# Linear attention, gated MLP and top-1 MoE on one core: the products with the state as eight half-column matmuls in place of four whole ones

## The chip, the core and the metric

The kernel runs on one core of a Trainium2 chip, in f32. The metric is the time of one execution on the device, in microseconds. The median of three runs of the kernel before is 538.46 us (538.27 to 538.58).

## What is computed

Three stages follow one another: a linear attention with a decaying state, a gated MLP, and a mixture of eight experts of which each token takes one. The change lies in the first.

```python
q, k, v: (2, 8, 768, 64)     # batch, heads, tokens, width; lam: one decay for each head
for b in range(nb):          # blocks of tokens, in order
    intra = einsum('bhic,bhjc->bhij', qb, kb) * Dmask      # scores, weighed by the decay
    intra = einsum('bhij,bhjd->bhid', intra, vb)
    inter = einsum('bhid,bhde->bhie', qb * lam_pow, kv_state)
    out[:, :, sl] = intra + inter
    kv_state = lam_block * kv_state + einsum('bhsd,bhse->bhde', kb * rev_pow, vb)
x = moe2(moe(out))
```

## The kernel before

The attention works on 12 tiles (n = 0 to 11, NT = 12), each 128 tokens of one of the two batches, in turn: even n are batch 0, odd n batch 1. The eight heads stand as four pairs (NPAIR = 4); the two heads of a pair (z = 0, 1) take partitions 0 to 63 and 64 to 127.

TensorE's instructions for a tile are four blocks, written out in order by the loop at L836:

- `from_state(n)`, for n of 2 and more: four matmuls (L792), one for each pair. The stationary operand is the pair's state, 128x128, in which only the two 64x64 blocks on the diagonal hold values and the others are zero. The moving operand is `qs`, the queries times powers of the decay, 128x128. The product starts the sum in the output bank. It waits for `qs` (POOL), for the state (VectorE) and for `xl_ready`, with which VectorE gives the bank free.
- `to_state(n)`, for n from 1 to 9: eight matmuls (L808) with the decayed keys `kd` as 128x64 stationary, the output in partitions z*64 to z*64+63.
- `scores(n + 1)`: eight matmuls (L783), 64 rows by 128 columns.
- `within(n)`: eight matmuls (L819) with 128x64 stationary (values) and 128 moving columns (`pt`, the weighed scores). They add to the output bank and write partitions z*64 to z*64+63, pair by pair.

Around them: the SyncE queue loads a tile's input in two transfers (L456, L457) once `within(n - 4)` is done. POOL makes `kd` (L590), `qs` (L601) and `faded`, the decayed state (L606). VectorE weighs the scores into `pt` (L1667), splits the output into a high and a low part (`xh` by ScalarE at L1246, `xl` by VectorE at L1607), and adds to the state (L1686). From n = 8 on it also makes a difference of tiles, `xt` (L1737). ScalarE copies the output as `xt` and `xh`, and splits the first MLP weights (`gvh`). In tile 11 VectorE makes `gvl` (L1693) straight behind the weighing; the first product of the MLP, `gate_val(0, 0)` (L857), waits for it. From there TensorE runs the MLP (L857, L865, L889, L932) and the experts (L1159, L1169).

In the profile each f32 matmul of the source is two weight loads and two matmuls, so the four matmuls of `from_state` are x8 and the eight of the others x16.

Of the kernel before, what the change touches and what calls it, by code (L numbers as in the profile page):

```python
# [20 lines left out]
B, H, S, D = 2, 8, 768, 64  # L21
# [3 lines left out]
CH = 128  # L25
# [69 lines left out]
def bass_linear_attention_mlp_moe(nc, attn_in, lam_rows, mlp_w, router_w, expert_w, out):  # L95
    ctx = ExitStack()
    with ctx:
        def sb(name, shape, dt=F32, stack=ctx):
            return stack.enter_context(nc.sbuf_tensor(name, shape, dt))
# [62 lines left out]
        qs = [sb(f"qs{i}", [P, NPAIR, CH], F32, region1) for i in range(2)]  # L162
        kd = [sb(f"kd{i}", [P, H, D], F32, region1) for i in range(2)]
        pt = [[sb(f"pt{i}_{z}", [P, NPAIR, CH], F32, region1) for z in range(2)] for i in range(2)]
        state = [sb(f"state{b}", [P, NPAIR, P], F32, region1) for b in range(B)]
# [65 lines left out]
        bank = ctx.enter_context(nc.psum_tensor("bank", [P, 8, 512], F32))  # L231
# [122 lines left out]
        S_BANK, O_BANK, K_BANK = (0, 4), (2, 6), (3, 7)  # L354
# [85 lines left out]
        def read_passes(eng):  # L440
            eng.wait_ge(slots_ready, 1)
            return eng.value_load(passes[0:1, 0:1], min_val=1, max_val=MAXPASS)
# [328 lines left out]
        def _(pe):  # L771
            mm = nc.tensor.matmul
# [14 lines left out]
            def from_state(n):  # L787
                pe.wait_ge(qs_ready, n - 1)
                pe.wait_ge(state_ready, 2 * (n - 1))
                pe.wait_ge(xl_ready, n - 1)  # L790
                for a in range(NPAIR):
                    last = mm(bank[:, O_BANK[n % 2], a * CH:(a + 1) * CH], state[n % 2][:, a, :], qs[n % 2][:, a, :],  # L792
                              start=(a == 0), stop=False, skip_group_check=True)
                last.then_inc(inter_done, 1)

            def to_state(n):
# [39 lines left out]
            for n in range(NT):  # L836
                if n >= 2:
                    from_state(n)
                if 1 <= n < LAST_STATE:
                    to_state(n)  # L840
                if 1 <= n < NT - 1:
                    scores(n + 1)
                within(n)
# [390 lines left out]
            n = read_passes(pe)  # L1234
# [947 lines left out]
```

## Time and profile before

| what | value |
|---|---|
| median of three runs | 538.46 us (538.27 to 538.58) |
| the profiled execution | 538.59 us |
| its span, first to last instruction | 536.9 us |
| TensorE's granted clock, mean | 0.998 |
| TensorE busy | 528.0 us, 98% |
| VectorE, ScalarE, POOL busy | 352.4, 247.4, 75.4 us |
| attention, as far as the first product of the MLP | 0 to 51 us |

The profile is of one execution. Busy time of TensorE counts overlapping records, so the length of a block of matmuls is read from the start of the block to the start of the next one, or from the chain of work that ended last.

### The profile page before, as it was taken

What the parts mean: (1) busy time and instruction counts of PE and PEld (TensorE: products, weight loads), DVE (VectorE), ACT (ScalarE), POOL (GpSimd) and SP (SyncE); (2) the same over time, 40 slices, a digit from 0 to 9 for tenths busy, and PEclk for the clock granted to TensorE, in tenths of its full rate; (3) what the DMA queues carried; (4) which work ended last, traced back from release to release, by engine and by line L of the source; (5) the groups of instructions that cost most, each with busy time, mean ns of one, the idle gap of its engine ahead of it and who ended that gap; (6) DMA issues with size and microseconds to landing.
All of it is one profiled execution on the core that took longest, in us unless ns stands there. A gap on an engine that the chain in (4) does not pass through costs nothing.

```text
span 536.9 us, 8448 instructions
## 1 busy us (share of the span) xinstructions
PE 528.0 (98%) x3195; PEld 448.0 (83%) x3195; DVE 352.4 (66%) x609; ACT 247.4 (46%) x414; POOL 75.4 (14%) x94
## 2 busy tenths in 40 slices
PE   8999999999999999999999999999999999999995
PEld 7888888888888887887888888778999999999994
DVE  7779888795865647644556676567676666766620
ACT  4225465645353424442435444366555555555521
POOL 4992000000000000010000120023021130311001
PEclk9999999999999999999999999999999999999999
DMA  8987404132130304546253656256675666655000
GB/s 291 326 268 280 155 20 157 38 120 104 54 117 21 107 13 153 197 123 248 85 159 106 228 173 247 90 190 238 223 258 211 205 221 225 216 196 175 0 28 36
DMA packets 22280, 84.55 MB, mean 158 GB/s; under 512 B 3804, under 2 KB 3804, under 8 KB 18656
## 3 DMA queue, kind: packets, MB, share of 16 engines
q1 hardware_dynamic: 17376, 71.35, 38.4%
q0 software_dynamic: 3712, 10.54, 5.5%
q10 hardware_dynamic: 1152, 2.13, 1.0%
q8 instruction: 25, 0.41, 0.3%
q14 instruction: 15, 0.12, 0.1%
HBM read 75.59 MB, written 10.53 MB: 160 GB/s over the span
## 4 chain that ended last, share of the span: by engine, by line
PE 95%; issue 1%; DMA 1%; POOL 1%; SPq 0%; POOLq 0%; ACT 0%; DVE 0%
PE bank L932 18%; PE bank L857 16%; PE bank L1159 14%; PE bank L1169 12%; PE bank L865 12%; PE bank L889 6%; PE bank L1073 2%; PE bank L1092 2%; PE bank L783 2%; PE bank L792 2%; PE bank L819 2%; PE bank L1148 1%; PE bank L808 1%; DMA stages<-attn_in 1%; PE bank L959 1%
## 5 line engine op out<-in xcount | busy, mean ns | idle before, releaser
L1607 DVE TENSOR_TENSOR ewl<-stages,ewh 128x1024 fp32r<-128x1024 f32 x50 | 60.8, 1223 | 16.4 <-ACT ewh L1246 15.9
L1246 ACT ACTIVATE ewh<-stages 128x1024 fp32r<-128x1024 f32 x50 | 52.3, 1056 | 0.2 <-DMA stages<-expert_w 0.2
L1552 ACT ACTIVATE ehh<-bank 128x256 fp32r<-128x256 f32 x48 | 18.5, 385 | 58.0 <-PE bank L1159 57.9
L636 POOL DMA_DIRECT2D stages<-expert_w x8 | 4.6, 574 | 260.7 <-DVE more_hl L1607 185.1
L1169 PE MATMUL bank<-ewl,ehh 128*128 128x512 f32 x96 | 37.8, 394 | 0.0
L1169 PE MATMUL bank<-ewh,ehl 128*128 128x512 f32 x96 | 37.7, 392 | 0.0
L1169 PE MATMUL bank<-ewh,ehh 128*128 128x512 f32 x96 | 37.5, 390 | 0.0
L1159 PEld LDWEIGHTS bank<-exh,ewh 128*128 128x128 f32 x224 | 33.2, 188 | 3.6
L1159 PE MATMUL bank<-exh,ewh 128*128 128x256 f32 x224 | 36.0, 283 | 0.0
L2090 DVE SCALAR_TENSOR_TENSOR ehl<-bank,ehh 128x256 fp32r<-128x256 f32 x48 | 20.3, 422 | 23.8 <-ACT ehh L1552 23.7
L1159 PE MATMUL bank<-exl,ewh 128*128 128x256 f32 x224 | 34.8, 278 | 0.0
L1159 PE MATMUL bank<-exh,ewl 128*128 128x256 f32 x224 | 34.7, 277 | 0.0
L857 PE MATMUL bank<-xh,gvh 128*128 128x512 f32 x128 | 34.4, 391 | 0.0
L857 PE MATMUL bank<-xh,gvl 128*128 128x512 f32 x128 | 34.2, 389 | 0.0
L857 PE MATMUL bank<-xl,gvh 128*128 128x512 f32 x128 | 34.2, 389 | 0.0
L651 POOL DMA_INDIRECT gx<-x_rows,idx x15 | 16.1, 1076 | 106.8 <-issue 86.6
L1159 PEld LDWEIGHTS bank<-exl,ewh 128*128 128x128 f32 x224 | 30.2, 189 | 0.0
L1159 PEld LDWEIGHTS bank<-exh,ewl 128*128 128x128 f32 x224 | 29.7, 188 | 0.0
L1246 ACT ACTIVATE c<-bank 128x512 f32<-128x512 f32 x30 | 17.9, 596 | 24.3 <-PE bank L932 24.3
L865 PE MATMUL bank<-hh,woh 128*128 128x512 f32 x72 | 28.7, 399 | 0.0
L857 PEld LDWEIGHTS bank<-xl,gvh 128*128 128x128 f32 x128 | 24.0, 188 | 5.0
L857 PEld LDWEIGHTS bank<-xh,gvl 128*128 128x128 f32 x128 | 24.0, 188 | 5.0
(291 smaller groups left out, 1248.4 us busy)
## 6 DMA issues: line engine op xcount, KB each, us to landing
stages<-expert_w SPq DMA_DIRECT2D x21, 1024.0 KB, 4.9
stages<-mlp_w SPq DMA_DIRECT2D x24, 768.0 KB, 4.5
stages<-attn_in SPq DMA_DIRECT2D x18, 512.0 KB, 5.4
stage<-expert_w SPq DMA_DIRECT2D x7, 1024.0 KB
stages<-expert_w POOLq DMA_DIRECT2D x8, 512.0 KB, 5.5
stage<-attn_in SPq DMA_DIRECT2D x6, 512.0 KB, 5.6
held<-c SPq DMA_DIRECT2D x12, 256.0 KB, 2.0
stages<-held SPq DMA_DIRECT2D x12, 256.0 KB, 2.8
```

What stands on the lines that cost most here:

```text
L651: nc.gpsimd.indirect_dma_start(out=dst[:, :], out_offset=None, in_=src, in_offset=bass.IndirectOffsetOnAxis(ap=at, axis=0), bounds_check=l ...
L783: last = mm(bank[:, S_BANK[n % 2] + z, a * CH:(a + 1) * CH], kt[z * D:(z + 1) * D, a, :], qt[z * D:(z + 1) * D, a, :], start=True, stop=True)
L857: last = mm(bank[:, where, :], wt[:, k, :], (xh, xl)[x][:, k, g * GT:(g + 1) * GT], start=(at == 0), stop=(at == 3 * KD - 1))
L865: last = mm(bank[:, d, :], (woh, wol)[w][wo][:, d * P:(d + 1) * P], (hh, hl)[x][h][:, :], start=(f == 0 and n == 0), stop=True, skip_group ...
L889: last = mm(bank[:, d, :], (woh, wol)[w][j % 3 + 1][:, d * P:(d + 1) * P], (hh, hl)[x][j % 3 + 1][:, :], start=(j == 0 and n == 0), stop=True,
L932: last = mm(where, mix(i, w)[:, n * KH * P + k * P:n * KH * P + (k + 1) * P], moving[i][x][:, k, :], start=(first and at == 0), stop=(at = ...
L1159: last = mm(bank[:, H_BANK + f % 2, 0:CAP], expert_bufs(par)[w][:, f, k * P:(k + 1) * P], (exh, exl)[z][par][:, k, :], start=(at == 0), st ...
L1169: last = mm(bank[:, Y_BANK + t, 0:DM], (ehh, ehl)[z][f % 2][:, t * P:(t + 1) * P], expert_bufs(par)[w][:, f, KD * P:], start=(f == 0 and n ...
L1246: return nc.scalar.activation(dst, src, ACT.Copy)
L1552: nc.scalar.activation(ehh[f % 2][:, :], bank[:, H_BANK + f % 2, 0:CAP], ACT.Relu).then_inc(ehh_ready, 1)
L1607: V.tensor_tensor(dst, src, high.bitcast(F32), ALU.subtract).then_inc(inc, 1)
L2090: V.scalar_tensor_tensor(out=ehl[f % 2][:, :], in0=bank[:, H_BANK + f % 2, 0:CAP], scalar=0.0, in1=ehh[f % 2][:, :].bitcast(F32), op0=ALU.max,
```

## The change

`from_state` makes each product as two matmuls. Half z takes columns z*64 to z*64+63 of the pair's state as a 128x64 stationary and writes partitions z*64 to z*64+63 of the output bank. The moving operand is the same 128 columns of `qs` for both. Start flags, waits and the semaphore on the last matmul are as before, and so are the results: each half still takes all 128 rows, zeros included.

```diff
                 for a in range(NPAIR):
-                    last = mm(bank[:, O_BANK[n % 2], a * CH:(a + 1) * CH], state[n % 2][:, a, :], qs[n % 2][:, a, :],
-                              start=(a == 0), stop=False, skip_group_check=True)
+                    for z in range(2):
+                        part = slice(z * D, (z + 1) * D)
+                        last = mm(bank[part, O_BANK[n % 2], a * CH:(a + 1) * CH], state[n % 2][:, a, part],
+                                  qs[n % 2][:, a, :], start=(a == 0), stop=False, skip_group_check=True)
                 last.then_inc(inter_done, 1)
```

## Rows read from the trace of the kernel before

**Rows 1.** The page: TensorE's busy time, and the chain's shares by engine
```profile
PE 528.0 (98%) x3195; PEld 448.0 (83%) x3195; DVE 352.4 (66%) x609; ACT 247.4 (46%) x414; POOL 75.4 (14%) x94
...
PE 95%; issue 1%; DMA 1%; POOL 1%; SPq 0%; POOLq 0%; ACT 0%; DVE 0%
```

**Rows 2.** The chain in order of time: start us, us, what; attention and beyond
```profile
26.59 1.09 PE bank L792 x8
...
29.39 1.02 PE bank L819 x16
...
51.00 21.98 PE bank L857 x96
```

**Rows 3.** Waits of PE, whole run: engine line, releaser: us, times, longest
```profile
PE bank L792 <- POOL qs L601: 0.5, 1, 0.5
PE bank L1202 <- DVE ewl L2106: 0.3, 1, 0.3
```

**Rows 4.** Single lines of PE: ns min/median/max, first and last start, forms
```profile
L792 PE MATMUL bank<-qs,state x80: 275/275/377, 15.1 to 49.7; 128*128 128x128 f32 x80
...
L819 PE MATMUL bank<-pt,stages x144: 272/273/323, 11.0 to 48.6; 128*64 128x128 f32 x144
```

**Rows 5.** Timeline of PE, a tile in the middle: start us, us, instructions
```profile
23.79 0.69 PE L808 MATMUL bank<-stages,kd 128*64 128x64 f32 x16
24.40 1.16 PE L783 MATMUL bank<-stages 64*128 64x128 f32 x16
25.50 1.09 PE L819 MATMUL bank<-pt,stages 128*64 128x128 f32 x16
26.52 1.16 PE L792 MATMUL bank<-qs,state 128*128 128x128 f32 x8
```

**Rows 6.** Timeline of PE, the first tiles, where L808 and L819 are neighbours
```profile
10.96 1.05 PE L819 MATMUL bank<-pt,stages 128*64 128x128 f32 x16
11.83 0.63 PE L808 MATMUL bank<-stages,kd 128*64 128x64 f32 x16
12.40 1.16 PE L783 MATMUL bank<-stages 64*128 64x128 f32 x16
```

**Rows 7.** Timeline of all engines: `qs` of tiles 3 and 5, from_state of tile 3
```profile
16.98 1.19 POOL L601 TENSOR_TENSOR qs<-stage,powers 128x512 f32<-128x512 f32 x1
...
18.88 1.16 PE L792 MATMUL bank<-qs,state 128*128 128x128 f32 x8
...
23.42 1.18 POOL L601 TENSOR_TENSOR qs<-stages,powers 128x512 f32<-128x512 f32 x1
```

**Rows 8.** Issue of tile 8's second load, landing of these loads, scores(8)
```profile
27.00 0.43 SPq L457 DMA_DIRECT2D stages<-attn_in  x1
...
DMA to landing us min/median/max: 4.0/5.1/6.8
...
35.86 1.16 PE L783 MATMUL bank<-stages 64*128 64x128 f32 x16
```

**Rows 9.** Stretches: us, busy of five engines, PEclk, DMA share, GB/s
```profile
15.06:18.95 3.89, 3.89 (x57) 3.41 (x57) 3.36 (x7) 0.68 (x2) 3.89 (x4) 1.00 0.98 355
26.59:30.41 3.82, 3.82 (x57) 3.34 (x57) 2.73 (x6) 1.09 (x2) 3.82 (x5) 1.00 0.81 278
```

**Rows 10.** Timeline of ScalarE and VectorE, tiles 8 to 11
```profile
41.91 0.60 ACT L1246 ACTIVATE xt<-bank 128x512 f32<-128x512 f32 x1 [3.22 <-PE bank L819]
...
45.26 1.29 DVE L1667 TENSOR_TENSOR pt<-bank,decay 128x512 f32<-128x512 f32 x2
...
47.98 1.29 DVE L1667 TENSOR_TENSOR pt<-bank,decay 128x512 f32<-128x512 f32 x2 [0.24 <-PE bank L783]
49.19 1.22 DVE L1693 TENSOR_TENSOR gvl<-stages,gvh 128x1024 fp32r<-128x1024 f32 x1
```

**Rows 11.** Timeline of PE, the first product of the MLP
```profile
50.93 1.20 PE L857 MATMUL bank<-xh,gvh 128*128 128x512 f32 x4
```

**Rows 12.** Timeline of VectorE during the first MLP products
```profile
67.58 0.69 DVE L1779 TENSOR_TENSOR hid<-bank,sig 128x512 f32<-128x512 f32 x1 [0.74 <-PE bank L857]
```

## The prediction

> **What bounds the kernel now.** I read the page first: the TensorE row of part 1 is busy for 98% of the span and the chain that ended last is 95% TensorE [rows 1]. So time taken off TensorE's stream is worth its full size, unless something else is nearly as late. Then the chain in order of time, over the attention. From tile 3 on it never leaves TensorE before the MLP's first product, and it repeats four blocks for each tile: from_state (L792) for 1.09 us, to_state (L808), scores (L783), and within (L819) for 1.02 us [rows 2]. The middle two are read from starts in the timeline, 0.61 and 1.10 [rows 5]; together 3.82 us. The waits of TensorE over the whole run hold only one that touches the changed line, 0.5 us for `qs` at the first from_state [rows 3]. So the questions are how long the new block takes, what it does to the blocks beside it, and who is late next.
>
> **How long a block is, and what a change of shape costs.** The answers for single lines give the shapes [rows 4]: L792 is 128 rows by 128 columns, L819 is 128 by 64; the timeline has L808 with 128 by 64 and L783 with 64 by 128 [rows 5]. Each f32 matmul has two records, so from_state has 8 now and will have 16 with exactly the shape of L819 (128x64 stationary, 128 columns streamed). In the repeating pattern a block's length is the distance of two starts. L819 takes 25.50 to 26.52, that is 1.02, with another shape before and behind it [rows 5]. The trace has one place where L819 stands between two L808 blocks, all of 128x64: there it takes 10.96 to 11.83, 0.87 us [rows 6]. So 16 records of this shape cost 0.87 (0.109 for a pair of halves), and the two changes of shape around L819 cost 0.15. They can be parted. L808 at 23.79 takes 0.61 with a change ahead and one behind; at 11.83, with none ahead, it takes 0.57 [rows 5, 6]. Entering this shape thus costs 0.04 to 0.05 (starts are rounded to 0.01; I take 0.05), and leaving L819 for another one costs the other 0.10.
>
> The Trainium skill (TensorEngine Tiling (Array Packing), Key Properties) says that changing the tiling mode, not just the tile, drains the engine; the trace agrees, and by it the new order has two drains for each tile in place of four.
>
> **The change part by part.** It removes four whole matmuls and adds eight halves, in ten blocks (n = 2 to 11). I call this profile's clock of 1.00 unchanged: TensorE stays dense.
> 1. The block itself, between L819 and L808, costs 0.87 in place of 1.09: 0.22 less [rows 2, 6].
> 2. The L819 ahead of it no longer changes shape at its end: 0.10 less, 0.92 in place of 1.02. L808 behind it no longer changes shape at its start: 0.05 less, 0.57 in place of 0.61 to 0.62.
> 3. So a tile of the pattern is 0.87 + 0.57 + 1.10 + 0.92 = 3.46 in place of 3.82, 0.36 less. This holds for n = 3 to 9: 7 x 0.36 = 2.52.
> 4. n = 2 starts when `qs` is there, so only its own 0.22 and L808's 0.05 count: 0.27. In n = 10 scores follow: 0.87 + 0.10 = 0.97 in place of 1.09, and 0.10 ahead: 0.22. In n = 11 both neighbours are L819: 0.10 + 0.22 + 0.05 = 0.37.
> The sum is 0.27 + 2.52 + 0.22 + 0.37 = 3.38 us of TensorE's time. The semaphore on the last matmul, the number of waits and their order stay; nothing is moved past a queue. Four instructions more in the source are 8 more records in a block, which I cost inside the 0.87, since L819's 16 are issued at that pitch.
>
> **Who is late next.** POOL: `qs` of n = 3 ends at 16.98 + 1.19 = 18.17 [rows 7], and the block that needs it starts at 18.88 and would start at 18.88 - 0.36 = 18.52. Cover 0.35. Later it grows: for n = 5 `qs` ends at 23.42 + 1.18 = 24.60, its block starts at 26.52 [rows 5] and would start 3 x 0.36 = 1.08 earlier, with 0.84 left. So nothing is paid. Loads: a tile's two transfers are issued once within(n - 4) is done, the second at 27.00 for n = 8; the longest landing of any is 6.8 us, so by 33.8, and scores(8) start at 35.86, 2 us later [rows 8]. At a shorter tile the issue moves up too, but three tiles pass between: the cover falls by about 3 x 0.36 = 1.1 and stays positive. The mean rate must go from 278 to about 278 x 3.82 / 3.46 = 307 GB/s, and 355 was moved in the first stretch [rows 9]. Cost 0, and if the cover is gone, at most some tenths.
>
> VectorE is where a part comes back. The first gate product (L857 at 50.93) needs `gvl`, which VectorE makes behind the last weighing. Follow it from the end of within(8), where ScalarE starts at 41.91: two copies, then on VectorE `xl`, two `state` adds, `xt`, `pt` at 45.26, `xl`, `xt`, then `pt` at 47.98 after an idle 0.24 that TensorE's scores ended, then `gvl` at 49.19 to 50.41 [rows 10]. That chain is 8.50 us with 0.24 of waiting for TensorE: it can't be shorter than 8.26, and 0.05 for the signal makes 8.31. TensorE takes 50.93 - 41.91 = 9.02 for the same stretch [rows 11]. All gains of n = 9, 10 and 11 lie in it, 0.36 + 0.22 + 0.37 = 0.95, so it would want `gvl` after 8.07. It waits 0.24 us. Its first part is hidden in a short wait for `pt` ahead of the last within. Bounds: 0 (if the VectorE steps pack tighter) and 0.5 (if ScalarE's copies or the load of the first weights also come later than I think).
>
> Behind this point the first 96 records of L857 run to 72.98 [rows 2], and VectorE idles among them, waiting for results of L857 itself, here for 0.74 us [rows 12], so it is tied to TensorE and moves with it. The longest wait of TensorE later in the run is 0.3 us [rows 3]. I carry the gain to the end.
>
> The net is 3.38 - 0.24 = 3.14 us. The profiled execution took 538.59 us (its span 536.9 and 1.7 around it), so 535.45; the median of the three runs is 538.46, so 535.3.
>
> **The rivals.**
> A. Slower: the two halves do not run side by side. Both have all 128 rows and stream the same `qs`, which no pair in this trace does (L819 streams two `pt` tiles). If each of 16 records then took the 0.109 of a pair, the block is 1.74 us, the tile 1.74 + 0.57 + 1.10 + 0.92 = 4.33 in place of 3.82, and ten of them cost about 5 us: 543.5. It decides from the pair's pitch: above (0.87 + 0.36) / 8 = 0.154 us for a pair the change loses. Against it: L819 and L808 have 128 rows too and pair.
> The Trainium skill (TensorE: Matmul & The Clock Gate, Part 3, The mechanism) says that a weight load overlaps matmuls in flight only if its row group differs. Here both halves hold the same rows, and by that rule this rival would come; the 0.87 us for 16 records of L819 already speaks against it [rows 6].
> B. No change that can be measured: the cost at a block's edge comes with the new line's operands and waits, not with the shape. Then the new block is like L819 with its edges, 1.02 in place of 1.09, ten times 0.07: 537.8. Against it: the 10.96 block changes operands and line too and pays nothing.
> C. Half of it: another engine comes late over the middle tiles (POOL's `qs` at n = 3 with its cover of 0.35, the loads, or a longer wait for `gvl`). 1 to 2 us of the gain go: 536.8.
>
> **How the numbers follow.** Chances: the forecast 0.76, C 0.10, B 0.06, A 0.08. What a measurement of this kernel can tell from no change is about 0.2%, 1.1 us. Faster by more: 0.76 and nearly all of C, 0.85. Within it: B and a rest of C, 0.07. Slower: 0.08. The forecast's own ends are 3.38 + 0.2 (rounding of the block lengths, 10 x 0.02) at 534.8 and 3.38 - 0.5 at 535.6; to hold C's better half the range goes to 536.6, and to 534.7 below.
>
> **What would show it.** In the profile after: L792 with x16 in a block, its records 128x64 with L819's duration (273 ns), a block of 0.87 and a tile of 3.46; L808 at 0.57 and L819 at 0.92; from_state(11) starting 3.0 us or so earlier, and the first L857 about 3.1 us earlier, with the wait for `gvl` in TensorE's list. L792 blocks over 1.2 us mean A, 1.02 means B, waits for POOL or DMA in the tiles mean C. The prediction fails as a whole if TensorE waits after 51 us for something that was just in time.

## The result, and the profile after

The changed kernel takes 535.73 us (median of 6 runs, 535.25 to 536.08) against 538.46 (538.24 to 538.80): a ratio of 0.9949, 95% interval 0.9938 to 0.9960. That is 2.7 us less, inside the range, 0.4 above the predicted 535.3. The profiled execution took 536.05 us with a span of 534.3, 2.6 shorter than the span before.

The chain of work that ended last, in order of time (start us, us, what), first a tile in the middle, then the end of the attention:

```profile
25.59 0.87 PE bank L794 x16
26.46 0.46 PE bank L810 x16
26.93 1.09 PE bank L783 x16
28.02 1.02 PE bank L821 x16
29.04 0.87 PE bank L794 x16
...
37.34 0.42 DVE state L1688
37.75 0.03 issue
37.78 0.43 DVE state L1688
38.21 0.03 issue
38.24 0.21 DVE xt L1739
38.45 1.57 issue
40.02 0.58 DVE pt L1669
```

Lines behind the change have moved by two: L794 is from_state, L810 to_state, L821 within, L859 the first gate products. Against [rows 2] the block of from_state is 0.87 in place of 1.09, and it has 16 records. (The chain cuts the edge between L794, L810 and L821 otherwise than the timeline does; the sum of the four is the tile either way, 3.45.) The new thing is the second part. Before, the chain stayed on TensorE to the MLP; now it goes over VectorE from 37.3 to 47.1 us, and in it stand 1.57 us in which `xt` was at work on nothing that the profile shows.

The timeline of TensorE (start us, us, engine, line, operation, count):

```profile
22.84 0.63 PE L810 MATMUL bank<-stages,kd 128*64 128x64 f32 x16
23.40 1.16 PE L783 MATMUL bank<-stages 64*128 64x128 f32 x16
24.50 1.09 PE L821 MATMUL bank<-pt,stages 128*64 128x128 f32 x16
25.42 1.04 PE L794 MATMUL bank<-qs,state 128*64 128x128 f32 x16
26.29 0.64 PE L810 MATMUL bank<-stages,kd 128*64 128x64 f32 x16
...
43.66 1.16 PE L783 MATMUL bank<-stage 64*128 64x128 f32 x16
44.88 1.09 PE L821 MATMUL bank<-pt,stages 128*64 128x128 f32 x16
45.78 1.07 PE L794 MATMUL bank<-qs,state 128*64 128x128 f32 x16
47.28 1.10 PE L821 MATMUL bank<-pt,stage 128*64 128x128 f32 x16 [0.43 <-DVE pt L1669]
48.37 1.17 PE L859 MATMUL bank<-xh,gvh 128*128 128x512 f32 x4
```

Read by starts, as [rows 5] was: L821 0.92 in place of 1.02, L794 0.87 for 1.09, L810 0.56 for 0.61, L783 1.10 as before. Each is within 0.01 of its prediction. At the end L794 stands at 45.78 and L821 only at 47.28, 1.50 later where 0.87 is the block: 0.63 us of waiting for `pt`, of which the row names 0.43 (the rest is the tail of the matmuls before). Two smaller waits stand around it: L783 takes 43.66 to 44.88, 1.22 where 1.10 is its length, and L821 takes 47.28 to 48.37, 1.09 where 0.97 is (0.87 for the block and 0.10 for leaving its shape). That is 0.12 each. Together 0.87 us.

I measure all runs below in one stretch, from the start of the first from_state to the start of the first L857 (L859 here): everything that the change can reach lies in it, and the start of the kernel, which varies by some tenths of a microsecond with the first loads, lies outside. Before it is 15.06 to 50.93, 35.87 us; after 15.01 to 48.37, 33.36. The gain is 2.51, which is the predicted 3.38 less those 0.87. What follows is the same within the 0.1 us to which the spans are given: 486.0 us before (50.93 to 536.9) and 485.9 after (48.37 to 534.3).

### The profile page after: what moved, and what is told of

Read it like the earlier page. It is cut to its first block, busy times and chain, and to the rows that moved or that the text cites. A ratio compares the mean times of both kernels' runs of the same rounds, so it can differ in the third digit from the quotient of the medians.

```text
span 534.3 us, 8608 instructions
## 1 busy us (share of the span) xinstructions
PE 525.4 (98%) x3275; PEld 447.9 (84%) x3275; DVE 353.3 (66%) x609; ACT 247.1 (46%) x414; POOL 74.4 (14%) x94
## 4 chain that ended last, share of the span: by engine, by line
PE 95%; issue 2%; DVE 1%; POOL 1%; POOLq 0%; ACT 0%
PE bank L934 18%; PE bank L859 16%; PE bank L1161 15%; PE bank L1171 12%; PE bank L867 12%; PE bank L891 6%; PE bank L1075 2%; PE bank L1094 2%; PE bank L783 2%; PE bank L821 1%; PE bank L794 1%; PE bank L1150 1%; PE bank L829 1%; PE bank L961 1%; PE bank L1204 1%
## 5 line engine op out<-in xcount | busy, mean ns | idle before, releaser
L859 PE MATMUL bank<-xh,gvh 128*128 128x512 f32 x128 | 34.4, 391 | 0.0
L859 PE MATMUL bank<-xh,gvl 128*128 128x512 f32 x128 | 34.2, 389 | 0.0
L859 PE MATMUL bank<-xl,gvh 128*128 128x512 f32 x128 | 34.2, 389 | 0.0
L859 PEld LDWEIGHTS bank<-xh,gvl 128*128 128x128 f32 x128 | 24.0, 188 | 5.0
L859 PEld LDWEIGHTS bank<-xl,gvh 128*128 128x128 f32 x128 | 24.0, 188 | 5.0
```

The lines of the kernel that those rows point to most:

```text
L859: last = mm(bank[:, where, :], wt[:, k, :], (xh, xl)[x][:, k, g * GT:(g + 1) * GT], start=(at == 0), stop=(at == 3 * KD - 1))
```

## Experiments

**The changed kernel once more**, for a second profile.

> The changed kernel once more, for its profile. Theory (the long xt is a meeting of VectorE and POOL that depends on a few tenths of a microsecond): the stretch from the first from_state to the MLP is again over 32.7, with xt of tile 8 between 0.69 and 1.75, and the time 535.7 within 0.3. Rival (the long xt was an accident of one profile): xt 0.69 and a stretch of 32.7.

The median was 536.01 us, the ratio 0.9954 (0.9941 to 0.9968), the stretch 15.10 to 48.28, 33.18 us. The long `xt` is there again. The timeline of VectorE and POOL in the changed kernel:

```profile
37.25 1.05 POOL L606 TENSOR_TENSOR faded<-state,powers 128x512 f32<-128x512 f32 x1
...
38.24 1.75 DVE L1739 TENSOR_TENSOR xt<-xt 128x512 f32<-128x512 f32 x1
38.26 1.18 POOL L601 TENSOR_TENSOR qs<-stages,powers 128x512 f32<-128x512 f32 x1
...
42.72 0.69 DVE L1739 TENSOR_TENSOR xt<-xt 128x512 f32<-128x512 f32 x1
```

The same in its second profile:

```profile
38.19 1.17 POOL L601 TENSOR_TENSOR qs<-stages,powers 128x512 f32<-128x512 f32 x1
...
38.33 1.57 DVE L1739 TENSOR_TENSOR xt<-xt 128x512 f32<-128x512 f32 x1
```

`xt` ends at 39.99 and 39.90; POOL's `qs` of tile 10 at 39.44 and 39.36. The two stretches differ by 0.18 us, as the two `xt` do. In the first, `xt` was issued while `faded` still ran, to 38.30, and `qs` went ahead of it. Both times `xt` ends 0.54 to 0.55 us behind the end of `qs`, and its own work is 0.69: it ran when POOL let go, shortly ahead of its recorded end. That this is what happened is so far argued from two rows. Before the change `xt` began at 40.70 and `qs` had ended at 40.46, so they missed one another by 0.24 us:

```profile
39.28 1.18 POOL L601 TENSOR_TENSOR qs<-stages,powers 128x512 f32<-128x512 f32 x1
...
40.70 0.69 DVE L1737 TENSOR_TENSOR xt<-xt 128x512 f32<-128x512 f32 x1
```

VectorE's `xt` moved up by 2.46 us with the shorter tiles, POOL's `qs` only by 1.02. They shifted against each other by 1.44 us, and 0.24 would have been enough.

**POOL's `qs` held back, then POOL's decay held back.** The first run moves the operation that met `xt`, the second keeps POOL idle during the first two `xt`.

```diff
@@ qs_held: queries(n)
                 if n >= 4:
                     pool.wait_ge(inter_done, n - 3)
+                if n == 10:
+                    pool.wait_ge(turn_ready, 1)
@@ fade_held: queries(n), fade(n)
+                if n == 11:
+                    pool.wait_ge(turn_ready, 2)
...
                 pool.wait_ge(state_ready, 2 * (n - 1))
+                if n == 9:
+                    pool.wait_ge(turn_ready, 1)
```

> The changed kernel with one wait more: POOL makes qs of tile 10 only after VectorE's first difference xt. Theory (that xt took 1.75 us in place of 0.69 because POOL's qs of tile 10 was running beside it): it takes 0.69, and of the 0.87 us of stall some 0.6 go, so 535.1 to 535.2. Rival (the 1.75 us has nothing to do with POOL): xt stays long in some runs, 535.7.

> The changed kernel with two waits on POOL: the decay of the state for tile 9 comes only after VectorE's first difference xt, and qs of tile 11 only after the second, so that nothing of POOL runs beside either. Theory (an xt, which reads both operands from SBUF, can't start beside a POOL operation and ends 0.69 us after that one): all xt take 0.69, the stretch from the first from_state to the first MLP product takes 32.5 to 32.7 us, the time is 535.1 to 535.4. Rival (something else stretched the first xt, such as the transfers or ScalarE): it still takes over 1 us, the stretch is over 32.7.

With `qs` held, `xt` met POOL's `faded`, the operation before, and again ended 0.55 behind it. The timeline of VectorE, POOL and TensorE in that run:

```profile
37.55 1.05 POOL L608 TENSOR_TENSOR faded<-state,powers 128x512 f32<-128x512 f32 x1
...
38.09 1.06 DVE L1741 TENSOR_TENSOR xt<-xt 128x512 f32<-128x512 f32 x1
...
39.31 1.19 POOL L603 TENSOR_TENSOR qs<-stages,powers 128x512 f32<-128x512 f32 x1 [0.72 <-DVE xt L1741]
...
45.52 1.04 PE L796 MATMUL bank<-qs,state 128*64 128x128 f32 x16
46.47 1.09 PE L823 MATMUL bank<-pt,stage 128*64 128x128 f32 x16
47.57 1.16 PE L861 MATMUL bank<-xh,gvh 128*128 128x512 f32 x4
```

With POOL idle there, all four took 0.68 to 0.69 (the answer for the tile, `xt`: ns min/median/max):

```profile
L1743 DVE TENSOR_TENSOR xt<-xt x4: 680/687/693, 38.1 to 48.4; 128x512 f32<-128x512 f32 x4
```

The transfers went on beside the first of them (a DMA share of 0.85, against 0.92 beside the long one). ScalarE does not stretch it either: it was idle during the `xt` of 1.06 us, and busy for 0.51 us of the changed kernel's second `xt`, which took 0.69. So the cause is POOL's operation. The expectation of `qs_held` was wrong in one part, that `xt` would be 0.69: 1.06 remained, with another partner. The stretches were 14.85 to 47.57, 32.72 us, and 14.88 to 47.65, 32.77: 0.64 and 0.59 less than the changed kernel's first profile (0.46 and 0.41 less than its second). What waiting is left in `qs_held` can be read off the last rows: 0.95 for a block of 0.87 and 1.10 for one of 0.97, 0.21 in all. The medians were 535.50 us (ratio 0.9940, 0.9927 to 0.9953) and 535.48 (0.9948, 0.9935 to 0.9962). These intervals overlap with that of the changed kernel, so the profiles show a shorter attention, but the times do not show a faster kernel. Both medians lie above what was expected, by 0.3 and 0.1 us.

The Trainium skill (SBUF — State Buffer, SBUF: two separate sides) says that a VectorE operation with two inputs in SBUF and a GpSimd operation that reads SBUF exclude each other for a whole instruction. The trace agrees: `xt` has both inputs in SBUF and took 1.57 and 1.75 us, while `state`, `pt` and `xl`, with one input from PSUM, ran beside POOL at their usual length (`pt` 1.29 for two).

`fade_held` took 0.37 us more off the first `xt` than `qs_held` and yet did not get below it, nor into the expected 32.5 to 32.7: the next thing is ready hardly sooner. ScalarE's row in this run:

```profile
45.22 1.06 ACT L1252 ACTIVATE gvh<-stages 128x1024 fp32r<-128x1024 f32 x1 [1.86 <-DMA stages<-mlp_w]
```

It waited 1.86 us for the first MLP weights, and `gvl` needs `gvh`, so `gvl` began at 46.32. In `qs_held` it was nearly the same: `gvh` ended at 46.20 and `gvl` began at 46.24. The trace before shows no wait of ScalarE there.

**The differences moved away from VectorE's tiles.** Two ways, each on both kernels. In the first VectorE makes them later; in the second POOL makes them behind its last `qs`.

```diff
@@ late_turns, late_turns_before (vector)
-                if n >= NT - 4:
-                    turn(1, n - (NT - 4))
             split_out(0, 0)
             tokens_low(NT - 1)
             split_mlp(0, 1)
+            for t in range(4):
+                turn(1, t)
@@ turns_pool, turns_pool_before (gpsimd; vector leaves them out, and waits for turn_ready 4 ahead of turn(0, 0))
+            for t in range(4):
...
+                nc.gpsimd.tensor_tensor(xt[:, at, :, 2 * P:4 * P], xt[:, x, :, 2 * P:4 * P], xt[:, y, :, 2 * P:4 * P],
+                                        ALU.subtract).then_inc(turn_ready, 1)
```

> The changed kernel with the four differences of tiles (xt, turn(1, t)) taken out of VectorE's tiles 8 to 11 and made behind the first MLP weights. Theory (TensorE gained 3.38 us and VectorE's chain in tiles 8 to 11 took back 0.87): the stretches ahead of within(10), within(11) and the first MLP product close, so about 538.46 - 3.4 = 535.1, 0.6 below the changed kernel. Rival (the blocks of matmuls themselves are slower there): 535.7, with the same gaps.

> The kernel before with the same move of the four differences. Theory: nothing was late there, so no change, 538.5 (within 0.2). Rival (VectorE's load in these tiles cost something before too): faster by 0.3 or more.

> The changed kernel with the four differences xt of tiles 8 to 11 made by POOL behind its last qs, so that VectorE has nothing of them and nothing is put off to where the MLP needs VectorE. Theory (VectorE's chain costs the changed kernel 0.87 us, and putting the differences off cost 1.8 behind the attention): the stretch from the first from_state to the first MLP product takes 32.5 us (35.87 - 3.38), or up to 32.9 if the load of the first weights ends last, in place of 33.36; the rest of the run stays 485.9. Time 535.1 to 535.5. Rival (a difference on POOL gets in VectorE's way as much): 535.7 or more.

> The kernel before with the same move of the differences to POOL. Theory: nothing was late there, the stretch stays 35.87 us and the time 538.5. Rival (VectorE's differences cost before too): a shorter stretch, faster by 0.3 or more.

The stretch and what follows it to the end of the span, from the starts in each profile:

| run | stretch, us | rest of the span, us | time, us | ratio (95%) |
|---|---|---|---|---|
| before | 35.87 | 486.0 | 538.46 | |
| changed | 33.36 | 485.9 | 535.73 | 0.9949 (0.9938 to 0.9960) |
| late_turns | 32.87 | 487.8 | 536.85 | 0.9971 (0.9960 to 0.9982) |
| late_turns_before | 35.87 | 487.5 | 539.93 | 1.0025 (1.0016 to 1.0034) |
| turns_pool | 33.10 | 485.9 | 536.54 | 0.9965 (0.9952 to 0.9979) |
| turns_pool_before | 35.87 | 486.0 | 538.86 | 1.0002 (0.9993 to 1.0011) |

The stretch of the kernel before doesn't move, whoever makes the differences: VectorE was covered there. In the changed kernel it moves at once. So VectorE's chain is what takes back part of the gain, and only since the change.

It is not the only thing. Free of its differences, VectorE still did not bring `late_turns` to 32.49, which is 35.87 less the 3.38. There the load of the first MLP weights is last. The chain of this run, and its timeline of VectorE:

```profile
39.05 5.98 DMA stages<-mlp_w
...
46.15 1.23 DVE L1695 TENSOR_TENSOR gvl<-stages,gvh 128x1024 fp32r<-128x1024 f32 x1 [0.32 <-ACT gvh L1248]
```

The load is issued behind within(8) and took 5.98 us. In the kernel before it was issued at 41.91 and ScalarE began with the weights at 46.36, at most 4.45 later. So `gvl` waits for `gvh`, and the stretch holds 0.38 us more than the sum of TensorE's blocks.

As better kernels both failed, against what I expected. `late_turns` was to win 0.6 us and lost 1.1. Waits of TensorE over its whole run:

```profile
PE bank L859 <- DVE sig L1774: 1.7, 1, 1.7
```

Four differences in a row put off VectorE's next step, `sig`, for which TensorE then waits 1.7 us in the MLP (1.3 in `late_turns_before`, which lost 1.35 us against the kernel before). I had looked at VectorE's idle time over the whole of the first products, not at what stands next in its queue. In `turns_pool` POOL's last difference met `gvl`, which has both inputs in SBUF too:

```profile
45.68 1.86 DVE L1704 TENSOR_TENSOR gvl<-stages,gvh 128x1024 fp32r<-128x1024 f32 x1
...
41.11 5.35 POOL L624 TENSOR_TENSOR xt<-xt 128x512 f32<-128x512 f32 x4
```

1.86 us in place of 1.22 [rows 10] is the same exclusion at another pair. In `turns_pool_before` `gvl` took 1.47, and in both runs it ends 1.08 us behind POOL's last difference; in the kernel before there was room for it. Without the 0.64 us that `gvl` grew by, the stretch of `turns_pool` would be 32.46, by this estimate the whole of the 3.38. Its profiled execution took 535.24 us but the five ranged up to 537.18. Which of them lost what is open, since the one that was profiled is the fastest.

**Halves that are not neighbours.** The loops of from_state changed over, four lower halves and then four upper ones.

```diff
-                for a in range(NPAIR):
-                    for z in range(2):
+                for z in range(2):
+                    for a in range(NPAIR):
```

> The changed kernel with the loops in from_state changed over: the four lower halves, then the four upper ones, so that no two neighbours lie in different column halves. Theory (the 0.87 us come from neighbours in different columns running side by side, 0.109 for a pair): each record then takes about 0.1 by itself, a block some 1.7 us, ten of them 8 us more: about 543.5. Rival (a half is simply half as long, whatever its neighbour): no change, 535.7.

539.98 us, ratio 1.0028 (1.0019 to 1.0037): slower than before the change, by 1.5 us. It has the same instructions and the same shapes as the changed kernel and is 4.3 us behind it, so it is the side-by-side pair that pays. (In the changed kernel the two neighbours also stream the same `qs`, and here they don't; but L819 streams two different `pt` tiles and has its 16 records in 0.87 us too [rows 6].) The expected 543.5 was too high. The timeline of TensorE shows why:

```profile
26.61 1.20 PE L794 MATMUL bank<-qs,state 128*64 128x128 f32 x13
27.55 0.27 PE L810 MATMUL bank<-stages,kd 128*64 128x64 f32 x1
27.65 0.27 PE L794 MATMUL bank<-qs,state 128*64 128x128 f32 x1
...
27.76 0.27 PE L794 MATMUL bank<-qs,state 128*64 128x128 f32 x1
...
27.87 0.27 PE L794 MATMUL bank<-qs,state 128*64 128x128 f32 x1
```

The chain of the same run has `from_state`'s first records of another tile:

```profile
30.72 0.32 PE bank L794 x3
```

Three records in 0.32 us are 0.107 for each, as expected of a half alone; but the last upper halves ran between and beside the first matmuls of to_state, which lie in the lower columns. TensorE does not need the partner to be the very next one. The same goes on inside the block: its first 13 records start within 0.94 us, where one after another, at 0.107, they would need 1.3. Tile 10, where scores follow and not to_state, shows it by itself:

```profile
46.31 1.53 PE L794 MATMUL bank<-qs,state 128*64 128x128 f32 x16
47.77 1.16 PE L783 MATMUL bank<-stage 64*128 64x128 f32 x16
```

Here the block takes 1.46 us, of which 0.10 is for leaving the shape; 16 halves one after another would take 1.7, in pairs they take 0.87. A tile was 3.94 us (22.67 to 26.61) in place of the 4.33 that rival A had.

**A change of shape taken away without halves.** The kernel before, with scores ahead of to_state.

```diff
-                if 1 <= n < LAST_STATE:
-                    to_state(n)
                 if 1 <= n < NT - 1:
                     scores(n + 1)
+                if 1 <= n < LAST_STATE:
+                    to_state(n)
```

> The kernel before (whole matmuls) with scores(n + 1) ahead of to_state(n), so that to_state and within, both 128x64, are neighbours: three changes of shape for a tile in place of four. Theory (a change of shape costs 0.15 with its entry and exit, whatever the lines are): a tile takes 3.67 in place of 3.82, nine tiles give 1.3 us, so 537.2, less what VectorE's state adds lose by coming later in tiles 8 to 11. Rival (the edge costs nothing by itself, and the gain of the change came from the halves): 538.5.

537.73 us, ratio 0.9986 (0.9977 to 0.9995). The chain:

```profile
22.34 1.09 PE bank L792 x8
23.43 1.09 PE bank L783 x16
24.52 0.61 PE bank L808 x16
25.14 0.88 PE bank L819 x16
26.01 1.09 PE bank L792 x8
```

A tile is 3.67 us, exactly 0.15 less than 3.82, with whole matmuls. The stretch, 14.93 to 50.09, is 35.16, only 0.71 less than before: eight tiles of 0.15 would be 1.20. In tiles 8 to 11 the chain goes over VectorE here too, since the state adds come later, and TensorE waits for `pt` (timeline):

```profile
49.00 1.09 PE L819 MATMUL bank<-pt,stage 128*64 128x128 f32 x16 [0.21 <-DVE pt L1667]
```

So the pair of edges costs the same 0.15 at other lines, and a second edit ran into the same second bottleneck.

## Why the prediction came out as it did

**The terms for TensorE were right.** The block was predicted at 0.87 and measured at 0.87, within at 0.92 and 0.92, to_state at 0.57 and 0.56 to 0.57, the tile at 3.46 and 3.45. With `qs_held` the stretch shrank by 3.15 us, and it still holds the 0.21 of waiting read there: 3.36, against 3.38 in the sum. How it splits: `scores_first` shows that each pair of edges is worth 0.15 a tile without any halves, and `halves_apart` that the 16 records need their neighbours in the other columns.

**VectorE as the next one late was right, its size was not.** The mis-sized term is the wait of 0.24 us. TensorE's stretch lost 3.38 - 2.51 = 0.87 in the first profile and 3.38 - 2.69 = 0.69 in the second. The chain that I followed from 41.91 on was the right one, but I took its lengths, and its start, over from the trace before. The `xt` two steps ahead of the first VectorE step in it became 1.06 longer, because the shorter tiles moved VectorE up against POOL by 1.44 us. With that `xt` shortened or put right the loss is 3.38 - 3.15 = 0.23 (`qs_held`) and 3.38 - 3.10 = 0.28 (`fade_held`), as the prediction had it, though in `fade_held` it is the load of the first weights as much as VectorE. Part of this agreement is luck: in `qs_held` the chain took 8.16 us from ScalarE's start (39.30 to 47.46) where I had 8.26, and from the end of `gvl` to TensorE's start it was 0.11 where I had put 0.05 from no row. My upper bound of 0.5 for this wait named ScalarE's copies and that load, not an operation that grows: the bound was too tight. By the bounds of this sum the time would have been 535.6 at most (its lower end should read 534.9, not 534.8), and 535.73 lies above; it is inside the range because that was widened for C.

**The covers of POOL and of the loads held in the tiles.** In the changed kernel TensorE waits for POOL only at the first from_state, and for no load in tiles 3 to 11. The one load whose cover went was the first of the MLP, where ScalarE now waits (1.25 us in the changed kernel). It costs nothing as long as VectorE is later; in `late_turns`, where VectorE is not, it costs 0.38 us. I had counted the covers of the attention's loads, and of this one only said that it might come later.

**The rivals.** A (the halves don't pair) did not come, and the rule of the Trainium skill that I cited for it (TensorE: Matmul & The Clock Gate, Part 3, The mechanism) does not describe these halves: they hold the same rows, and 16 records took 0.87 us. Its price of 5 us was not met: the version that parts the halves lost 1.5, as halves of different columns still overlap in part there. B (the edges belong to the lines) is refuted by `scores_first`. C is what happened in part: 0.6 us beyond the forecast wait went to another engine over the last tiles, though through a meeting of VectorE and POOL and not through any cover that I had counted.

## What to carry to other kernels

When neighbours of a block of matmuls are half-column products, making the block half-column too can pay even though it doubles the instructions: look for the place in the trace where two such blocks already touch, and read both the block's length and the price of the edge from it. Write the two halves of a pair next to one another. Then recount the second engine over the whole stretch with its steps shifted against each other, and mark the operations with both inputs in SBUF that could now fall on a POOL operation that reads SBUF; an engine that was covered in every tile can set the end after a gain of 0.36 us a tile.

## What the runs showed of the hardware that I had not expected

- A VectorE operation with both inputs in SBUF waits for a running POOL operation and the wait is recorded as its own duration: `xt` took 1.75, 1.57 and 1.06 us in place of 0.69, and `gvl` 1.86 and 1.47 in place of 1.22 in `turns_pool` and `turns_pool_before`. It ends 0.14 us less than its own usual length behind POOL's operation (0.55 for 0.69, 1.08 for 1.22). The profile shows no releaser; only the row of POOL beside it tells.
- TensorE overlaps half-column matmuls of different columns although others stand between them in the program, and even across the edge of two blocks: in `halves_apart` a record of to_state began at 27.55 while from_state had three of its own still to start.
